# Attention and two expert layers in one kernel: the first loads reordered, and TensorE multiplying ones while it waits

## What is computed

```python
# 1. attention, 16 heads (2 batches x 8), 768 tokens, width 64; proj is [64, 6]
q_bits = einsum(q, proj) > 0                      # 6 hash bits for each token
k_bits = einsum(k, proj) > 0
mask = bucket(q_bits)[:, None] == bucket(k_bits)[None, :]
scores = where(mask, q @ k.T / 8, -1e9)           # only tokens of the same bucket see each other
x = softmax(scores) @ v
# 2. dense expert layer: 8 experts, all tokens, gates balanced by 8 Sinkhorn steps
x = sum_e P[:, e] * (relu(x @ w1[e]) @ w2[e])     # w1[e] 512x1024, w2[e] 1024x512
# 3. routed expert layer: each token that is not skipped goes to its best expert
x = x + gate * (relu(x @ w1b[e]) @ w2b[e])
```

## Time and profile before

| | |
|---|---|
| median of 3 runs | 1343.03 us (1342.31 to 1348.64) |
| profiled execution | 1345.64 us, of which the span is 1343.8 us |
| TensorE busy | 1314.8 us, 98% of the span |
| TensorE weight loads busy | 760.6 us, 57% |
| DVE, ACT, POOL busy | 843.8, 565.9, 289.2 us |
| DMA | 109.84 MB, mean 82 GB/s |

### The profile page before, as it was taken

The page is one execution under the profiler, slowest core; times in us unless marked ns, Lnnn a source line. Parts: engine busy times, 40 slices in busy tenths (PEclk is TensorE's granted clock), DMA queues, the critical chain, the costliest instruction groups (busy, mean ns, idle before and its releaser), DMA issues.

```text
span 1343.8 us, 24739 instructions
## 1 busy us (share of the span) xinstructions
PE 1314.8 (98%) x9435; PEld 760.6 (57%) x9435; DVE 843.8 (63%) x1487; ACT 565.9 (42%) x868; POOL 289.2 (22%) x251
## 2 busy tenths in 40 slices
PE   6999999999999999999999999999999999998997
PEld 3676677655455456445545644554564455556675
DVE  5999999796576237426624743663474265567994
ACT  5999999642134114304411430431143043225762
POOL 3667666622001100300200030020003000121111
PEclk9999999999999999999999999999999999999999
DMA  9344451051011011001101100110110023368960
GB/s 238 95 112 114 101 121 39 33 205 63 1 63 64 1 63 62 0 0 62 62 0 62 62 0 0 62 62 0 62 62 0 5 71 120 125 208 291 325 227 21
DMA packets 51632, 109.84 MB, mean 82 GB/s; under 512 B 5216, under 2 KB 8840, under 8 KB 51568
## 3 DMA queue, kind: packets, MB, share of 16 engines
q1 hardware_dynamic: 48880, 105.40, 24.7%
q0 software_dynamic: 2240, 3.35, 0.7%
q10 hardware_dynamic: 448, 0.19, 0.1%
HBM read 93.57 MB, written 17.34 MB: 83 GB/s over the span
## 4 chain that ended last, share of the span: by engine, by line
PE 91%; DVE 4%; ACT 1%; issue 1%; DMA 1%; SPq 1%; POOL 0%; ACTq 0%; POOLq 0%; DVEq 0%
PE ps L1674 14%; PE ps L1678 14%; PE ps L1677 14%; PE ps L1700 11%; PE ps L1703 11%; PE ps L1702 11%; PE ps L1597 5%; PE ps L1585 2%; PE ps L1587 2%; PE ps L1569 2%; PE ps L1607 1%; PE ps L1609 1%; PE ps L1611 1%; DVE rh_lo L1500 1%; DVE w_lo L1191 1%
## 5 line engine op out<-in xcount | busy, mean ns | idle before, releaser
L1700 PE MATMUL ps<-x_hi,w_hi 128*128 128x384 f16 x896 | 292.1, 326 | 1.9 <-DVE parts L1254 1.1
L1703 PE MATMUL ps<-x_hi,w_lo 128*128 128x384 f16 x896 | 292.1, 326 | 0.0
L1702 PE MATMUL ps<-x_lo,w_hi 128*128 128x384 f16 x896 | 292.1, 326 | 0.0
L1678 PE MATMUL ps<-w_hi,h 128*128 128x512 f16 x768 | 291.0, 379 | 0.0
L1677 PE MATMUL ps<-w_lo,h 128*128 128x512 f16 x768 | 291.0, 379 | 0.0
L1674 PE MATMUL ps<-w_hi,h 128*128 128x512 f16 x768 | 291.0, 379 | 0.0
L1311 DVE SCALAR_TENSOR_TENSOR x<-ps,gate_now,x 128x512 f32<-128x512 f32 x84 | 63.1, 751 | 251.7 <-PE ps L1678 250.8
L927 ACT ACTIVATE x1s<-ps 128x384 f32<-128x384 f32 x64 | 30.4, 475 | 327.3 <-PE ps L1703 327.3
L625 POOL TENSOR_TENSOR wf<-wf 128x1024 f32<-128x1024 f32 x8 | 18.8, 2354 | 633.2 <-PE ps L1703 622.5
L944 ACT ACTIVATE h<-parts 128x1152 f16<-128x1152 f32 x64 | 74.4, 1163 | 142.3 <-DVE parts L1269 142.3
L1678 PEld LDWEIGHTS ps<-w_hi,h 128*128 128x128 f16 x768 | 75.1, 98 | 90.6
(11 more groups left out here) (228 smaller groups left out, 2234.3 us busy)
## 6 DMA issues: line engine op xcount, KB each, us to landing
wf<-w1a SPq DMA_DIRECT2D x32, 512.0 KB, 5.9
w_stage_in<-w2a SPq DMA_DIRECT2D x8, 2048.0 KB, 8.7
w_in<-w1b SPq DMA_DIRECT2D x4, 2048.0 KB, 9.6
w_in<-w2b SPq DMA_DIRECT2D x4, 2048.0 KB, 10.3
w_in_b<-w1b SPq DMA_DIRECT2D x4, 2048.0 KB, 10.5
w_in_b<-w2b SPq DMA_DIRECT2D x4, 2048.0 KB, 10.3
rows<-blank SPq DMA_DIRECT2D x1, 6682.0 KB, 21.5
qk_in<-kT SPq DMA_DIRECT2D x32, 192.0 KB, 4.2
```

The lines of the kernel that those rows point to most:

```text
L1678: last = pe.matmul(acc, a_lo, b_hi, start=False, stop=(m == n - 1))
L1700: pe.matmul(group_bank(g, role), w_hi, x_hi, start=(opens and kt == 0), stop=False, skip_group_check=not opens)
L1702: pe.matmul(group_bank(g, role), w_hi, x_lo, start=False, stop=False, skip_group_check=not opens)
L1703: last = pe.matmul(group_bank(g, role), w_lo, x_hi, start=False, stop=(kt == 1), skip_group_check=not opens)
```

## The change

1. DMAs. The second half of `proj` is loaded by SP, ahead of all its other loads, and no longer by ACT. The constants come in four pieces: 39 columns with the flags on ACT's queue, the identity on SP's queue behind the first q, the two other pieces on SP's queue behind the loads of head 1. V of head 0 is loaded ahead of the stack of head 1.
2. The load of the first w1 is moved from ahead of the loop over pairs to a place inside its first turn: behind the loads of head 2, ahead of `move_marks` of head 1. That turn is written out for it.
3. The `lo` part of k of head 0 is made by POOL and no longer by DVE. DVE makes `hash_bias` ahead of `first_buckets`.
4. ACT makes the `hi` parts of head 1 in step 1 of the first pair, and no longer ahead of the first exponential. TensorE transposes tile 0 ahead of the second half of the hash of head 1. POOL makes the marks of head 1 ahead of the `lo` part of its k.
5. TensorE multiplies 128x128 ones by 384 columns of ones into a bank that nobody reads: 12 times ahead of the first hash, 14 times ahead of the first scores, 4 times ahead of the scores of tile 2.

```diff
+            sp.wait_ge(zeroed, 1)
+            sp.dma_start(proj2[64:P, 32:32 + NBITS], proj).then_inc(proj_in, 16)
             load_stack(0, 0)
...
+            sp.dma_start(const[:, 0:P], consts[:, 0:P]).then_inc(consts_in, 16)
+            load_v(0, 0)
             load_stack(1, 1)
-            load_v(0, 0)
             load_qk(1, 1, 0)
             load_v(1, 1)
+            for cols in (slice(C_RANK, FLAGS.start), slice(FLAGS.stop, CONST)):
+                sp.dma_start(const[:, cols], consts[:, cols]).then_inc(ranks_in, 16)
             sp.dma_start(gates_in[:, :, :], gates).then_inc(gates_loaded, 16)
...
-            load_w1(w1_of[0])
-            with sp.Fori(1, G // 2) as j:
+            def load_pair(j, behind_even=lambda: None):
                 load_stack(2 * j, 0)
                 load_qk(2 * j, 0, j)
                 load_v(2 * j, 0)
+                behind_even()
                 move_marks(2 * j - 1, 1)
                 load_stack(2 * j + 1, 1)
                 load_qk(2 * j + 1, 1, j)
                 load_v(2 * j + 1, 1)
                 move_marks(2 * j, 0)
+
+            load_pair(1, lambda: load_w1(w1_of[0]))
+            with sp.Fori(2, G // 2) as j:
+                load_pair(j)
...
-            pool.wait_ge(q2_ready, 1)
+            split_k(0, 0)
             split_v(0, 0, 0)
-            pool.wait_ge(qk_lo, 2)
-            split_k(1, 1)
             pool.wait_ge(least_ready, 4)
+            pool.wait_ge(v_split, 3)
             mark_buckets(1, 0, None)
             pool.wait_ge(marks_ready, 1)
+            split_k(1, 1)
             split_q(1, 1)
...
-            act.dma_start(proj2[64:P, 32:32 + NBITS], proj).then_inc(proj_in, 16)
-            act.dma_start(const[:, C_RANK:CONST], consts[:, C_RANK:CONST]).then_inc(ranks_in, 16)
-            act.dma_start(const[:, 0:P], consts[:, 0:P]).then_inc(consts_in, 16)
+            act.dma_start(const[:, FLAGS], consts[:, FLAGS]).then_inc(flags_in, 16)
             act.wait_ge(first_k, 32)
...
-            split_k(1, 1, 0)
-            split_q(1)
...
                     if first and s in (0, 1):
                         take_hash(1, s)
+                    if first and s == 1:
+                        split_k(1, 1, 0)
+                        split_q(1)
...
+            def keep_busy(rounds):
+
+                for _ in range(rounds):
+                    pe.matmul(psT[0][:, :].rearrange("p (a n) -> p a n", n=P), ones16[:, :],
+                              ones16[:, :].unsqueeze(1).to_broadcast([P, HALF // P, P]), start=True, stop=True)
+
+            keep_busy(12)
             pe.wait_ge(proj_ready, 2)
             for c in range(2):
                 hash_tokens(0, c, 0, 0, bank=first_bank(c))
+            keep_busy(14)
             scores(0, 0, 0, 0, 0, opening=True)
             scores(1, 0, 1, 1, 0)
             hash_tokens(1, 0, 1, 0)
+            keep_busy(4)
...
-                    if first and s == 0:
-                        hash_tokens(1, 1, 1, 0)
-                    elif first and s == 2:
+                    if first and s == 2:
...
                     turn(i, s % 2)
+                    if first and s == 0:
+                        hash_tokens(1, 1, 1, 0)
```

More of the change, by code:

```diff
@@ L96 @@
 CONST = C_NONE + 1
+FLAGS = slice(C_EARLIER + 64, C_EARLIER + 96 + NBITS + 1)
 def build(nc, qT, kT, v, proj, consts, gates, w1a, w2a, w1b, w2b, rows, out):
@@ L284, in build @@
         qk_loaded = [sem(f"qk_loaded{r}") for r in range(2)]
-        first_q, first_k, ranks_in = sem("first_q"), sem("first_k"), sem("ranks_in")
+        first_q, first_k, ranks_in, flags_in = sem("first_q"), sem("first_k"), sem("ranks_in"), sem("flags_in")
         moved_in = [sem(f"moved_in{r}") for r in range(2)]
@@ L567, in mark_buckets @@
                 pool.wait_ge(hash_taken, 2 * g)
-                pool.wait_ge(qk_lo, 2 * g + (2 if moves_before is not None else 1))
+                pool.wait_ge(qk_lo, 2 * g + (2 if moves_before is not None else 0))
                 if moves_before is not None:
@@ L1129, in normalise_last @@
                                   ).then_inc(x_ready, 1)
-            dve.wait_ge(ranks_in, 16)
+            dve.wait_ge(flags_in, 16)
             dve.wait_ge(least_ready, 2)
@@ L1134, in _ @@
             dve.tensor_scalar(least[K_MARKS, :], below_k[K_MARKS, :], SMALLEST, None, ALU.mult).then_inc(least_ready, 1)
-            dve.wait_ge(least_ready, 4)
-            for c in range(2):
-                first_buckets(c)
             dve.tensor_scalar(hash_bias[Q_MARKS, :], below_q[Q_MARKS, :], 0.5, Q_MASK, ALU.is_lt, ALU.mult
@@ L1141, in _ @@
                               ).then_inc(least_ready, 1)
-            dve.wait_ge(qk_hi, 1)
-            dve.tensor_tensor(K2[0][0:64, :], qk_in[0][0:64, 1, :], A[0][0:64, 1, :], ALU.subtract
-                              ).then_inc(qk_lo, 1)
+            dve.wait_ge(least_ready, 6)
+            for c in range(2):
+                first_buckets(c)
             dve.wait_ge(qk_hi, 2)
@@ L1272, in expert @@
                     if first and g == 2:
+                        dve.wait_ge(ranks_in, 32)
                         dve.tensor_copy(earlier16[:, :], const[:, C_EARLIER:C_EARLIER + P]).then_inc(setup_ready, 1)
@@ L1653, in pair @@
                         turn_x(TURNED_AT.index(s))
+                    if first and s == 2:
+                        hash_tokens(2, 0, 0, 1)
+                    elif not last and q in HASH_AT and not (first and s < 2):
+                        hash_tokens(2 * j + r + 2, HASH_AT[q][0], r, j + 1, HASH_AT[q][1])
+                    turn(i, s % 2)
                     if first and s == 0:
                         hash_tokens(1, 1, 1, 0)
-                    elif first and s == 2:
-                        hash_tokens(2, 0, 0, 1)
-                    elif not last and q in HASH_AT and not (first and s == 1):
-                        hash_tokens(2 * j + r + 2, HASH_AT[q][0], r, j + 1, HASH_AT[q][1])
-                    turn(i, s % 2)
                     if not (first and s == 0):
```

## The result

The change takes **1351.42 us** in the median of 12 runs (1348.23 to 1353.74). The kernel before, timed again in the same series, takes 1346.96 us in 12 runs (1342.31 to 1348.96). The ratio is 1.004, with a 95% interval of 1.003 to 1.0051: slower by some 4.5 us between the medians, about 0.4%, and not zero. The prediction was 1341.6 us and a gain of 1.45 us. Of the 9.8 us between it and the median, 3.9 are the reference itself: the three runs shown had their median at 1343.03, the twelve have it at 1346.96. The effect was missed by 5.9 us.

What follows compares the result with a forecast made beforehand. The prediction took TensorE to bound the kernel, waiting only in the opening. The opening's 4.2 us shrink to 1.45 because tile 6 waits until 28.8 for the moves: 1343.03 - 1.45 = 1341.6 us, range 1338.2 to 1344.8.

Steps and rivals of the forecast that it cites:

- What bounds the kernel: Whole kernel: TensorE, busy nearly all the time from 30 us on; it waits only in the opening.
- the opening: Start up to tile 4's scores: 4.2 us gained, exponential 2 at 19.1, tile 4's scores at 20.2 in place of 24.55.
- tile 6's due time: First scores of head 1: due at 26.0 in place of 30.26, were there no wait for the moves.
- the signs: Profile after: TensorE waits 2 to 3 us ahead of tile 6; V of head 2 lands under 11.0 us after issue, w1 over 10.1.
- the mechanism: At head 1: the moves queue behind w1, so tile 6 waits from 26.0 to 28.8, leaving 1.45 us of gain.
- rival C: Opening: the ones don't raise the clock, so tile 6 comes 1.0 us later and the time is 1344.0; chance 0.08.
- Rival A: At head 1: the moves are not held back, so the whole 4.2 us is gained, 1338.8; chance 0.16.
- The moves (...) add 0.6 at 235 GB/s: 28.8: At head 1: w1's last byte lands at 28.2, the moves' 135 KB take 0.6 us more, tile 6 starts at 28.8.
- These cost nothing: Later loads, head 3 on: they keep their place in time, w1 is wanted much later; no cost.
- Rival B: At tile 6: the stall lowers the clock, +1.65 us for some 3.3 us at half speed, 1343.2 in all; chance 0.12.
- the likeliest case: Whole kernel: the moves wait behind w1 and 1.45 us is gained, 1341.6 us, own range 1340.3 to 1342.9; chance 0.60.
- from there on TensorE sets the pace as before: Behind tile 6: TensorE paces the rest as before, and nothing of the 2.8 us of idling comes back.

Runs made afterwards that it cites:

- w1_behind_moves: The change, with w1 loaded behind the three moves of head 1 and not ahead of them; 1347.11 us, ratio 1.0005 to before.
- ones_at_tile6: The change, with 90 more products of ones by 128 columns ahead of the scores of tile 6; 1348.37 us, ratio 1.0018 to before.
- hold_head3: The change, with SP holding head 3's loads until the moves of head 1 have landed; 1349.87 us, ratio 1.0022 to before.
- change_again: The change unaltered, run once more for a second profile; 1351.7 us (5 runs), ratio 1.004 to before.
- no_ones: The change without its 30 products of ones; 1346.91 us, ratio 1.0003 to before.
- behind_v3_no_ones: The change without its products of ones and with w1 behind V of head 3, ahead of the moves of head 2; 1344.34 us, ratio 0.9985 to before.
- behind_no_ones: The change without its products of ones and with w1 behind the moves of head 1; 1347.54 us, ratio 1.0017 to before.
- change_ones128: The change with 128 products of ones by 128 columns in place of the 30 of 384; 1351.26 us (7 runs), ratio 1.0031 to before.
- before_again: The kernel before unaltered, run once more for a second profile; 1346.77 us (10 runs), ratio 1.0.

## Why the prediction was wrong

**Held.** What bounds the kernel; the opening (exponential 2 at 18.94 for 19.1, tile 4 at 19.98 for 20.2); tile 6's due time (25.90 in `w1_behind_moves`, which has no wait there, for 26.0); the signs, V of head 2 landing 5.8 us after its issue and w1 12.5; the mechanism, that the moves stand behind w1 in the queue and TensorE waits for them at tile 6; and rival C's failure, since the ones do raise the clock (in the change; in `ones_at_tile6` it fell again at 11.9). Rival A, moves that overtake w1, is refuted by 6.28 us of waiting; only another order of issue gives what it promised.

**The step that failed first: "The moves (...) add 0.6 at 235 GB/s: 28.8".** It measured 31.85, 31.12 and 32.26 in three kernels with the change's order and ones, 29.48 without the ones and 29.63 with head 3 held back. The step took the landing to be where the total of the bytes ends. For fifteen of the sixteen engines that is right: all but the last three of the moves' landings in the change are there by 28.66. But a wait for a DMA ends with its slowest engine, and one engine lands its share of w1 at 30.77, 3.2 us behind the 15th, and its shares of the moves at 31.13 to 31.76. In `hold_head3` it is 1.3 us behind and the wait ends at 29.6. The rest, 1.5 us in `change_again` and 2.2 in the change, comes from head 3's loads, which run meanwhile; with them held back it is gone. So the prediction's sentence on the later loads, "These cost nothing", failed too. That the packet of code makes the first 1.06 us of the delay is inferred: in the change an engine falls back while the packet runs, by the packet's length, and in `no_ones`, whose packet comes later, none falls back so far. The trace doesn't name the engine of a packet, and no run took away the packet alone.

The rule that the prediction took from the Trainium skill ("DMA: Bandwidth & Descriptors", section "Queues, rings and completion order") is of the order within one ring, and the trace agrees with it: the late landings of the moves come behind that of w1. The same section says that a single DMA is split over up to 16 rings; the prediction's sum had no term for one of them being late.

**Rival B was set against the likeliest case, and it belongs to it.** Forecast at 1.65 us for some 3.3 us at half speed; the clock was low for 6.8 us and it cost 2.3 (against `ones_at_tile6`). A wait of 2.8 us might also have brought it: in `hold_head3` and `no_ones`, tile 6 runs at 0.58 us after waits of 3.4 and 3.0, and the clock stays low for 3.4 and 6.8 us. So the longer wait alone doesn't explain the longer stretch.

**A term that no row of before could show.** The sum ends with "from there on TensorE sets the pace as before". In all profiles with just the 30 products of ones it does not: TensorE stands one to three times between 1280 and 1307 us with nothing to wait for, the longest time 1.1 to 1.4 us. (In the change, timeline of TensorE:)

```profile
1287.55 0.22 PE L1690 MATMUL ps<-xgT_hi,w_hi_a 128*128 128x128 f16 x1
1289.20 0.22 PE L1693 MATMUL ps<-xgT_lo,w_hi_a 128*128 128x128 f16 x1 [1.43 <-issue]
```

The kernels with 0, 120 or 128 extra pairs don't have it. So it isn't what the ones do but how far they push later code along: my reading is that the number of instructions decides where the code is cut into the blocks that are fetched. The packets of code speak for it. Behind each of these waits (14 of them, of 0.4 us and more, in seven profiles) TensorE goes on 2.2 to 2.8 us after a packet of code starts; in the change the packets start at 1286.80, 1297.86 and 1304.20, and TensorE goes on at 1289.20, 1300.10 and 1306.99. And early in the kernel the packets move with the number of TensorE's instructions: 29.24 without ones, 25.02 with 30 pairs, 12.33 and 28.46 with 128. Why a packet comes too late with 30 pairs and in time with 0, 120 or 128 isn't shown.

**The account.** Profile against profile, on the predicted span of 1342.3:

| | us |
|---|---|
| tile 6 at 31.85 in place of 28.8 | +3.05 |
| clock after the wait | +2.3 |
| issue waits 1.4 + 1.1 + 0.6 | +3.1 |
| sum | 8.45 |
| measured, 1351.9 - 1342.3 | 9.6 |

The rest, 1.15 us, is of the size of what a stretch of lower clock in the routed layer can cost. It comes behind the same two waits as in the earlier trace rows but lasts 6.8 us in place of 3.4, which is worth at most 1.7 (before, the clock was back at 0.99 by 1225 to 1226; in the change it is low from 1225.0 to 1231.8):

```profile
1228.00:1229.00 1.00, 1.00 (x13) 1.00 (x11) 1.00 (x2) 0.00 (x0) 0.78 (x1) 0.50 1.01 389
```

It is longer in `hold_head3`, `w1_behind_moves` and `behind_v3_no_ones` too and not in `change_again`, so I don't put it down to the change. In the medians the change loses 4.5 us, not 8.1. What is safe of the split is that leaving out the ones gives back 4.5 us and moving w1 behind the moves 4.3, and that each also touches the other's loss; they don't add up (`behind_no_ones` is no better than either). In the profiles, moving w1 brings the mark 6.4 us forward and shortens what is behind it by 0.6; leaving out the ones gives 1.8 and 4.0. What part of the 4.5 is which isn't settled in the medians. `change_ones128`, with no issue waits and still 1351.26, shows that these waits alone don't decide it.

## What to carry to other kernels

Before adding the gain of an earlier start, go down the issuing queue and ask of each small, urgent transfer what stands ahead of it: here the 2 MB had to go behind the moves and behind the next head's loads, and only then was the opening's lead kept (1344.34 us without the ones, 1343.49 with 128 narrow ones, against 1346.25 to 1346.53 before). Price a wait for a DMA by its slowest engine and by what runs beside it, and price a wait of TensorE with the clock that follows it. Filler products are not free even where they are hidden: they are instructions, so compare more than one count of them before you believe or blame them.

## What was unexpected of the hardware

- While one packet of code takes 1.05 us of one DMA engine, one of w1's 16 landings falls 1.06 us behind the others. The 2 MB then land up to 2.4 us later (12.5 us after issue, 10.1 without a packet in its way).
- 30 extra products ahead of 14 us bring idle times of up to 1.4 us at 1280 to 1307 us; 120 or 128 bring none.
- The clock also falls where TensorE isn't idle: at 300 us in `before_again` it is busy throughout, at 0.50, behind 3 us of products of 16 columns.
